# Attention, experts and a product on one core: the softmax division moved from the weights to the outputs, and a different start

## What is computed

```
scores = scale * q @ k.T ;  cum = cumsum(max(s, 0))
scores = where(causal, -1e9, scores + min(-(cum_i - cum_j), 0))
attn   = exp(scores - max(scores))
attn   = attn / (sum(attn) + 1e-9)
x      = attn @ v                       # then 1152 tokens x 512
```

## Time and profile before

| what | value |
|---|---|
| median of 3 runs | 1173.54 us (1171.92 to 1175.3) |
| the profiled execution, its own time | 1174.52 us |
| its span in the trace | 1172.7 us |
| TensorE busy over the span | 98%, 6152 matmuls |
| DVE, ACT, POOL busy | 35%, 24%, 10% |
| mean granted TensorE clock | 0.997 |

### The profile page before, as it was taken

The page is one execution under the profiler, slowest core; times in us unless marked ns, Lnnn a source line. Parts: engine busy times, 40 slices in busy tenths (PEclk is TensorE's granted clock), DMA queues, the critical chain, the costliest instruction groups (busy, mean ns, idle before and its releaser), DMA issues.

```text
span 1172.7 us, 15312 instructions
## 1 busy us (share of the span) xinstructions
PE 1148.6 (98%) x6152; PEld 1029.0 (88%) x6152; DVE 411.5 (35%) x819; ACT 282.2 (24%) x569; POOL 113.0 (10%) x104
## 2 busy tenths in 40 slices
PE   7888899999999999999999999999999999999998
PEld 4666788899989989998998998999899899999997
DVE  4766435332224133232322413322232333433422
ACT  2666321212203112121220312212031231232210
POOL 1998530000000000000000000000000000000000
PEclk9999899999999999999999999999999999999999
DMA  7454220111011021011102202101120120120001
GB/s 195 112 123 102 82 73 1 54 54 36 19 54 72 0 72 59 12 36 54 54 0 72 72 0 70 51 22 34 38 72 1 36 72 1 36 73 10 27 27 54
DMA packets 52537, 59.59 MB, mean 51 GB/s; under 512 B 31600, under 2 KB 31600, under 8 KB 52496
## 3 DMA queue, kind: packets, MB, share of 16 engines
q1 hardware_dynamic: 52496, 59.02, 16.8%
HBM read 56.61 MB, written 2.40 MB: 50 GB/s over the span
## 4 chain that ended last, share of the span: by engine, by line
PE 93%; DVE 3%; ACT 2%; issue 1%; SPq 0%; DMA 0%; DVEq 0%; ACTq 0%
PE bank L1130 16%; PE bank L1132 16%; PE bank L1131 16%; PE bank L1265 13%; PE bank L1267 13%; PE bank L1266 13%; PE bank L1115 2%; DVE pT L740 1%; ACT scores L480 1%; PE bank L1041 1%; DVE scores L696 1%; PE bank L1037 1%; PE bank L1096 1%; PE bank L1002 1%; PE bank L1204 1%
## 5 line engine op out<-in xcount | busy, mean ns | idle before, releaser
L1130 PE MATMUL bank<-xh,w1h 128*128 128x384 f32 x1056 | 354.9, 336 | 0.0
L1132 PE MATMUL bank<-xh,w1l 128*128 128x384 f32 x1056 | 353.2, 334 | 0.0
L1131 PE MATMUL bank<-xl,w1h 128*128 128x384 f32 x1056 | 353.2, 334 | 0.0
L1265 PE MATMUL bank<-w2h,hh 128*128 128x512 f32 x684 | 267.2, 391 | 0.0
L1267 PE MATMUL bank<-w2h,hl 128*128 128x512 f32 x684 | 266.5, 390 | 0.0
L1266 PE MATMUL bank<-w2l,hh 128*128 128x512 f32 x684 | 266.4, 389 | 0.0
L548 ACT ACTIVATE hh<-bank 128x384 fp32r<-128x384 f32 x192 | 94.4, 492 | 618.8 <-PE bank L1132 618.8
L1130 PEld LDWEIGHTS bank<-xh,w1h 128*128 128x128 f32 x1056 | 198.4, 188 | 1.1
L1131 PEld LDWEIGHTS bank<-xl,w1h 128*128 128x128 f32 x1056 | 198.5, 188 | 0.7
L1132 PEld LDWEIGHTS bank<-xh,w1l 128*128 128x128 f32 x1056 | 198.4, 188 | 0.0
L753 DVE SCALAR_TENSOR_TENSOR hl<-bank,hh 128x384 fp32r<-128x384 f32 x192 | 106.7, 556 | 246.8 <-ACT hh L548 246.8
(11 more groups left out here) (107 smaller groups left out, 558.4 us busy)
## 6 DMA issues: line engine op xcount, KB each, us to landing
stage<-in_moe_w SPq DMA_DIRECT2D x64, 512.0 KB, 3.5
bias<-cum_dram SPq DMA_DIRECT2D x14, 288.0 KB, 3.6
stage<-in_moe_w_a SPq DMA_DIRECT2D x12, 256.0 KB, 2.6
stage<-in_moe_w_b SPq DMA_DIRECT2D x12, 256.0 KB, 3.0
stage<-in_moe_w_out SPq DMA_DIRECT2D x12, 256.0 KB, 2.6
bias_tail<-cum_dram SPq DMA_DIRECT2D x16, 144.0 KB, 4.1
nat<-in_q SPq DMA_DIRECT2D x16, 128.0 KB, 3.9
nat<-in_k SPq DMA_DIRECT2D x16, 128.0 KB, 3.2
```

The source lines that it names most:

```text
L1130: pe.matmul(o, w1h[:, c, col:col + PART], high, start=(c == 0), stop=False)
L1131: pe.matmul(o, w1h[:, c, col:col + PART], low, start=False, stop=False)
L1132: ins = pe.matmul(o, w1l[:, c, col:col + PART], high, start=False, stop=(c == KC - 1))
L1265: pe.matmul(o, hh[:, n % 2, f, at], w2h[:, f, :], start=(f == 0), stop=False)
```

## The change

1. POOL no longer multiplies the exponentials. `transpose_p` waits for `exp_done`, not `norm_done`, so unnormalised weights are transposed and multiplied by v.
2. `add_eps` and `invert` run once per pair on all nine columns. `spread_recips(p-1, part)` then spreads the reciprocals on TensorE: it takes a column of them, broadcast to 64 columns, as the weights and the identity as the moving operand, into a bank of the ring. Part 0 (4 matmuls of 128 columns) stands after units 2 and 3 and ahead of `score(p, 2)`; part 1 (4 of 128, 2 of 64) stands after units 5 and 6 and ahead of `score(p+1, 0)`. `copy_spread` (ACT) copies it to `spread`.
3. `scale_x` (DVE) multiplies the attention output by `spread` into `scaled`; `high_x` (ACT) now copies from `scaled`, and `low_x` moves to POOL.
4. `RING` has the two new users, one after unit 3 and one after unit 6.
5. Pair 0's bias is made once, by two matmuls of 512 columns before `score(0, 0)`, and copied by ACT to `bias[0]`; the 8 bias matmuls inside `score_tiles` go, and its memset on POOL too.
6. Pair 0's keys are issued by ScalarE's queue, not SyncE's. Constants are made with fewer waits on DVE, and those that the mask needs are made after `cum_rows`. TensorE runs seven extra matmuls of `own_half` first. `bias` rows are loaded to 512 columns, not 576.

The core of the diff:

```diff
     for _p in range(PAIRS):
         RING += [("unit", _p, u) for u in range(4)]
+        RING.append(("spread", _p, 0))
         if _p + 2 < PAIRS:
             RING.append(("tail", _p + 2))
-        RING += [("unit", _p, u) for u in range(4, 8)]
+        RING += [("unit", _p, u) for u in range(4, 7)]
+        RING.append(("spread", _p, 1))
+        RING.append(("unit", _p, 7))
...
         sp.dma_start(s_rows[:, :], sf).then_inc(s_loaded, DMA)
-        load_qk(0)
+        load_nat(0, qf, 0, q_loaded)
         load_qk(1)
...
-            for t in range(3):
-                normalise(p, t)
+            if p > 0:
+                low_x(p - 1, 0)
...
+        def copy_spread(p, part):
+            lo, hi = QRANGE[part]
+            act.wait_ge(spread_mm, 2 * p + part + 1)
+            at_least(act, x_scaled, 2 * (p - 2) + part + 1)
+            copy(spread[p % 2][:, lo:hi], ring_bank("spread", p, part)[:, 0:hi - lo], spread_done)
+
         def high_x(p, g):
             lo, hi = QRANGE[g]
-            act.wait_ge(pv_mm[g], p + 1)
-            copy(xh[:, p * S + lo:p * S + hi], X_BANK[g][:, 0:hi - lo], x_hi)
+            act.wait_ge(x_scaled, 2 * p + g + 1)
+            copy(xh[:, p * S + lo:p * S + hi], scaled[:, lo:hi], x_hi)
...
                 copy_pT(p - 1, 3)
+                copy_spread(p - 1, 0)
...
                 copy_pT(p - 1, 5)
+                copy_spread(p - 1, 1)
                 copy_pT(p - 1, 7)
...
+        def scale_x(p, g):
+
             lo, hi = QRANGE[g]
-            dve.wait_ge(x_hi, 2 * p + g + 1)
+            dve.wait_ge(pv_mm[g], p + 1)
+            dve.wait_ge(spread_done, 2 * p + g + 1)
+            at_least(dve, x_lo, 2 * (p - 1) + g + 1)
+            dve.tensor_tensor(scaled[:, lo:hi], X_BANK[g][:, 0:hi - lo], spread[p % 2][:, lo:hi],
+                              ALU.mult).then_inc(x_scaled, 1)
...
-                if p == 0:
-                    for r in range(2):
-                        pe.matmul(S_BANK[first + r][:, col:col + n],
-                                  ident[0:HEADS, r:r + 1].broadcast_to([HEADS, PART]), cum_rows[:, 0:n],
-                                  start=False, stop=False)
...
+        def spread_recips(p, part):
+
+            z = p % 2
+            ring_free("spread", p, part)
+            bank = ring_bank("spread", p, part)
+            pe.wait_ge(rec_done, p + 1)
+            for n, t in enumerate((2 * part, 2 * part + 1)):
+                for r in range(2):
+                    c = column(t, r)
+                    ins = pe.matmul(bank[r * D:(r + 1) * D, n * PART:(n + 1) * PART],
+                                    recips[:, z, c:c + 1].broadcast_to([PART, D]), ident[:, :], start=True, stop=True)
...
+            ins.then_inc(spread_mm, 1)
...
+        pe.wait_ge(half_set, 4)
+        for i in range(WARM_UP):
+            pe.matmul(S_BANK[0][:, 0:PART], own_half[:, :], own_half[:, :], start=True, stop=True)
         pe.wait_ge(const_set, 1)
         for i in range(3):
             transpose_qk(0, i)
+        pe.wait_ge(cum_done, 1)
+        for r in range(2):
+            pe.matmul(S_BANK[2 + r][:, :], ident[0:HEADS, r:r + 1].broadcast_to([HEADS, PART]), cum_rows[:, 0:MAIN],
+                      start=True, stop=True).then_inc(first_bias_mm, 1)
         score(0, 0)
...
                 transpose_p(p - 1, 2)
                 transpose_p(p - 1, 3)
+                spread_recips(p - 1, 0)
             score(p, 2)
...
                 transpose_p(p - 1, 5)
                 transpose_p(p - 1, 6)
+                spread_recips(p - 1, 1)
             if not last:
                 score(p + 1, 0)
```

More of the change, by code:

```diff
@@ L25 @@
 SINKHORN_ROUNDS = 8
+WARM_UP = 7
 DMA = 16
@@ L91, in attention_experts_product @@
     small, _ = sb("small", [PART, 96], F32)
-    s_rows, _ = sb("s_rows", [HEADS, S], F32)
+    cum_rows, _ = sb("cum_rows", [HEADS, S], F32)
+    s_rows, at = sb("s_rows", [HEADS, S], F32)
     s_pos, _ = sb("s_pos", [HEADS, S], F32)
-    cum_rows, _ = sb("cum_rows", [HEADS, S], F32)
     zero_rows, _ = sb("zero_rows", [HEADS, S], F32)
+    scaled, at = sb("scaled", [PART, S], F32, at - 4 * S)
+    spread = [None] * 2
+    for z in range(2):
+        spread[z], at = sb(f"spread_{z}", [PART, S], F32, at)
     identb, _ = sb("identb", [PART, PART], BF16)
@@ L409, in spread_tail_queries, with low_x @@
                                ALU.mult).then_inc(bd_done, 1)
-        def normalise(p, t):
-            z = p % 2
-            for r in range(2):
[L414 to L422, removed]
+        def low_x(p, g):
+            lo, hi = QRANGE[g]
+            pool.wait_ge(x_hi, 2 * p + g + 1)
+            cols = slice(p * S + lo, p * S + hi)
+            pool.tensor_tensor(xl[:, cols], scaled[:, lo:hi], xh[:, cols].bitcast(F32), ALU.subtract).then_inc(x_lo, 1)
         def split_w1_first(i):
@@ L510, in _ @@
             high_qk(0, i)
+        for r in range(2):
+            act.wait_ge(first_bias_mm, r + 1)
+            copy(bias[0][:, r, :], S_BANK[2 + r][:, :], first_bias)
         for p in range(PAIRS):
             if p > 1:
-                act.wait_ge(eps_done, 2 * (p - 2) + 2)
+                act.wait_ge(eps_done, p - 1)
             exp_tile(p, 0, 0, 1)
@@ L679, in _ @@
                           ALU.mult).then_inc(cum_done, 1)
+        dve.tensor_scalar(identb[:, :], ramp[:, :], place_of[:, 0:1], None, ALU.is_equal).then_inc(const_set, 1)
+        dve.tensor_scalar(maskb[:, :], ramp[:, :], place_of[:, 0:1], MASKED, ALU.is_gt, ALU.mult).then_inc(const_set, 1)
+        dve.wait_ge(const_set, 3)
+        for r in range(2):
+            rows = slice(r * D, (r + 1) * D)
+            dve.tensor_copy(maskt[rows, :], maskb[rows, r * TAIL:(r + 1) * TAIL]).then_inc(const_set, 1)
         def low_qk(p, i):
@@ L1020, in ring_free @@
                 pe.wait_ge(tr_lo, 3 * p + 3)
+            elif kind == "spread":
+                pe.wait_ge(spread_done, 2 * p + u[0] + 1)
             elif u[0] in BY_DVE:
@@ L1097, in transpose_p @@
             ins.then_inc(pt_mm, 1)
+        def spread_recips(p, part):
[4 more added lines that the diff above has]
+            for n, t in enumerate((2 * part, 2 * part + 1)):
+                for r in range(2):
+                    c = column(t, r)
+                    ins = pe.matmul(bank[r * D:(r + 1) * D, n * PART:(n + 1) * PART],
+                                    recips[:, z, c:c + 1].broadcast_to([PART, D]), ident[:, :], start=True, stop=True)
+            if part == 1:
+                for r in range(2):
+                    rows = slice(r * D, (r + 1) * D)
+                    ins = pe.matmul(bank[rows, 2 * PART:2 * PART + TAIL],
+                                    recips[rows, z, TAIL_COLUMN:TAIL_COLUMN + 1].broadcast_to([D, D]),
+                                    ident[rows, rows], start=True, stop=True)
+            ins.then_inc(spread_mm, 1)
         def attend(p, g):
@@ L1185, in _ @@
         transpose_p(LAST, 3)
+        spread_recips(LAST, 0)
         hidden(0, 0, 2)
@@ L1191, in _ @@
         transpose_p(LAST, 6)
+        spread_recips(LAST, 1)
         hidden(0, 0, 4)
```

110 lines of the change are left out of this document (55 added, 55 removed).

## The result

| what | before | after |
|---|---|---|
| median | 1173.59 us (1171.92 to 1175.3, 4 runs) | 1210.21 us (1206.97 to 1211.98, 4 runs) |
| the profiled execution, its own time | 1174.52 us | 1206.97 us |
| its span | 1172.7 us | 1205.0 us |
| mean granted TensorE clock | 0.997 | 0.984 |

The ratio is 1.0309, with a 95% interval of 1.0282 to 1.0335: the change makes the kernel 36.6 us slower. The forecast was 1198, within 1180 to 1214.

What follows compares the result with a forecast made beforehand. The prediction took a loop of latencies over TensorE, ScalarE and VectorE, not GpSimd, as the bound before the change. Six iterations +27.0, last iteration and last pair +4.8, start -7.5: +24.3 us, giving 1198 us, range 1180 to 1214.

Steps and rivals of the forecast that it cites:

- The loop of latencies: Pair loop over TensorE, ScalarE and VectorE, not GpSimd: added work is paid in full, +4.5 us per iteration, period 18.7.
- the first place: First spreading, ahead of score(p, 2), waits for VectorE's copy of unit 2: +2.0 us more per iteration.
- Both waits: Ahead of each spreading: VectorE's copy of unit 2 adds +2.0 us, ScalarE's copy of unit 5 adds +2.4, per iteration.
- The start of the iteration: VectorE's multiply ahead of ScalarE's copy makes the copy of the next queries late: +0.3 us per iteration.
- the clock falls: Rival: in the loop a longer stretch without other matmuls drops TensorE's clock, 3 to 4 us per iteration; chance 0.19.
- The start: Before the loop: fewer bias matmuls (-6.2), keys sooner and shorter constants (-1.3), -7.5 us; at most 2 beyond.
- The -1.3 (0 to -2): At the start: keys and later SyncE loads come sooner, VectorE's constants are shorter; -1.3 us, between 0 and -2.
- The last iteration and the last pair: Loop's last iteration +1.5 us for spreading and a copy, last pair +1.9 and +1.4 at its two spreadings; +4.8 together.
- between the places: Between the two spreadings: VectorE's multiply needs no wait for `xh` before the split of the tails; -0.2 us per iteration.
- The third: Rival: GpSimd held the loop through `transpose_p`'s wait for normalised tiles, so the change is faster, 1169 or 1163 us; chance 0.15.
- The second: Rival: only one of the loop's two waits is paid, +2.3 us per iteration, 1185 us; chance 0.09.
- The fourth: Rival: the effects cancel, iterations at about +0.5 us, total 1173 us; chance 0.04.

Runs made afterwards that it cites:

- e5_filled: The changed kernel with 6 and 7 matmuls that nobody reads put into TensorE's two waits ahead of the spreading; 1197.64 us, ratio 1.0202.
- h1_start_only: The kernel before with points 5 and 6 of the change and nothing else; 1169.96 us, ratio 0.9965.
- h3_one_queue: `h2_start_loads` with the first keys issued on SyncE's queue again, as before; 1165.61 us, ratio 0.9924.
- e3_second_behind: The changed kernel with only the second spreading group moved behind score(p+1, 0) inside the pair loop; 1191.53 us, ratio 1.0152.
- e1_both_behind: The changed kernel with both spreading groups moved behind the scores they stood ahead of, inside the pair loop only; 1178.39 us, ratio 1.0037.
- e2_first_behind: The changed kernel with only the first spreading group moved behind score(p, 2) inside the pair loop; 1198.51 us, ratio 1.0215.
- e4_no_spread: The changed kernel without spreading matmuls and their copies, the outputs multiplied by ones, so the division is left out; 1167.69 us, ratio 0.9937.
- h2_start_loads: `h1_start_only` with pair 2's queries and keys loaded ahead of w1; 1165.11 us, ratio 0.9929.
- v2_late_loads: The changed kernel, first spreading behind score(p, 2) and copied by VectorE, second behind unit 7 (also in RING), pair 2's loads early; 1168.66 us, ratio 0.9959.
- h4_no_extra: `h2_start_loads` without the extra matmuls at the start (WARM_UP = 0); 1165.59 us, ratio 0.9924.

## Why the prediction came out as it did

**The loop of latencies: right, and shown.** The period at full clock is 18.42 (`e5_filled`), forecast 18.7. That two iterations of the changed kernel took 18.64 and 18.83 is no closer hit: each has a fall of the clock at the first place. From the start of the score there to VectorE's tile 3 they take 1.44 and 1.62 (115.38 to 116.82, 54.16 to 55.78), where the third iteration takes 1.23 (72.98 to 74.21), and these 0.2 and 0.4 are what they have above 18.42. Both waits stand where they were said to: 1.47 ahead of the first spreading, released by VectorE's copy (forecast 1.5), 1.77 ahead of the second, released by ScalarE's (1.8); VectorE's gap ahead of tile 3 is 1.87 (2). The spreading took 0.66 (0.7) and 0.85 from the first to the score behind it (1.0); by columns, the lower bounds of 0.58 and 0.73 were nearer than those by count. The experiments that move each group give 1.55 and 1.23 for the order alone.

**The start of the iteration: +0.3 was too much.** The product's output waits for VectorE, and ScalarE's copy of the queries starts 0.9 after it as forecast, but an iteration with the multiply and without the spreading is 0.1 longer. The two errors in the loop, 0.3 for 0.1 and 1.0 for 0.85, make up most of the 0.3 between 18.7 and 18.42.

**What was mis-sized: the clock.** The prediction took "the clock falls" as a rival that would replace the forecast, at 3 to 4 in each iteration that has it, 1205 for two and 1219 for six. It came in all six. The prediction named "the clock column shows 0.5 to 0.8 in every iteration" as a sign of being wrong, and it came true: around the six falls the column reads 0.60 (40 to 45), 0.71 (53 to 57), 0.62 (80 to 88), 0.51 (103 to 109.4), 0.66 (115 to 120) and 0.71 (142 to 147.8). What kept the total near is the price: the six iterations lost 10.8 to it in the profiled execution (0.2 to 3.3 each), not 21, since a fall at the first place costs 0.2 to 0.4 and one at the second lasted for only a part of the product in the sixth iteration (3.39, not 4.32). The median's 1210 lies between the rival's two numbers. The clock is worth 12.6 in the medians. The step that failed is the choice of a likeliest case without any fall, worth 12.6 that the sum has at nothing, though the rows of the last iteration showed one behind a stretch of the same making, only longer.

**The rest agrees partly by luck.** `e5_filled` ran in 1197.64 and the forecast was 1198, but its terms are not those of the sum. From the kernel before to `e5_filled` the spans grew by 22.0: the six iterations +25.2 (forecast 27.0), the last iteration and the last pair +1.7 (forecast 4.8), the earlier start of the first iteration -5.0 (forecast -7.5). The cost was put too high and the gain too high as well, and the two errors cancel in part.

**The start: -7.5 was -4.1**, as `h1_start_only` measures it alone (in the changed kernel the first iteration starts 5.2 earlier). The sum of what was removed was a little low (pair 1's first bias comes 8.5 earlier, forecast 7 to 8). The bound on it was put wrongly: the forecast let pair 2's keys cap the gain at 2 beyond 7.5; it is pair 2's queries that cap it, and below 7.5. The -1.3 (0 to -2) for the keys' queue and the constants has no sign of the queue in it: `h3_one_queue` runs without it in the same time.

**The last iteration and the last pair: +4.8 was +1.4.** The last pair gave +2.9 (forecast 3.3). The last iteration gave -1.5 (forecast +1.5), and two things are seen in it. Its product ran at full speed here (159.45 to 161.66), which is 2.1 less. The spreading stands in the stretch where the clock had fallen before, but that it kept the clock up is not shown: `e3_second_behind` has the same order of matmuls there and its product took 3.71, while `e1_both_behind` and `e2_first_behind` had 2.27. So the 2.1 may be luck of this execution. And VectorE no longer waits for `xh`: the forecast's -0.2 "between the places" is all of the wait there, since no split of tails stands behind it. In the kernel before, and in `e4_no_spread`:

```profile
123.63 0.42 DVE L746 TENSOR_TENSOR xl<-bank,xh 128x256 fp32r<-128x256 f32 x1 [1.16 <-ACT xh L464]
```

```profile
118.30 0.42 DVE L766 TENSOR_TENSOR scaled<-bank,spread 128x256 f32<-128x256 f32 x1
```

`e4_no_spread`, which does the same start as `h1_start_only`, is 2.3 faster than it in the medians. In the two profiled executions, 1.2 apart, its last iteration takes 12.55 against 14.50, with products of nearly the same length (3.52 and 3.68), and no other part gains more than 0.4.

**The rivals.** The third, that GpSimd held the loop, falls with `e4_no_spread`. The second, that only one wait is paid, falls with `e2_first_behind` and `e3_second_behind`, which add. The fourth falls with the result. The first, the falling clock, is what happened, beside the waits of the forecast and not in place of them.

**A step ahead of the start that stays open.** The forecast gave the extra matmuls no effect. It also named a rule of the Trainium skill, "TensorE: Matmul & The Clock Gate", section "What's actually happening", that activity releases the throttle, by which they could have one. In the changed kernel the bias matmuls took 3.77, as before, so there the rule is not borne out. In `h2_start_loads`, with the same extra matmuls, the transposes at 6.18 took 1.06 for eight records instead of 1.94, and the bias matmuls 2.65, as the rule would have it; then the clock fell:

```profile
6.00:8.00 2.00, 1.82 (x12) 1.37 (x13) 1.48 (x6) 1.16 (x3) 0.00 (x0) 1.00 0.77 167
8.00:10.00 2.00, 2.00 (x4) 0.34 (x2) 0.96 (x3) 0.70 (x2) 0.72 (x1) 0.65 0.60 137
10.00:12.00 2.00, 2.00 (x15) 1.56 (x14) 0.00 (x0) 0.60 (x1) 0.00 (x0) 0.50 0.70 172
```

So the same start runs in two ways, and the early speed was lost again on the way. Of the eleven kernels profiled with the extra matmuls, four ran fast there (bias matmuls of 2.38 to 2.65 in `e5_filled`, `h2_start_loads`, `h3_one_queue` and `v2_late_loads`) and seven took 3.77 to 3.78, as did `h4_no_extra`, which has none. Over the runs it is worth nothing (1165.59 without). What decides which of the two it is was not settled.

## What to carry to other kernels

Before giving idle engines less to do, see whether anything waits for them: an engine at 10 of 10 us whose period stays the same at 7.6 of 10 is not the bound, and work put elsewhere to relieve it is paid on the loop that is. In an in-order engine the place of a wait costs more than the instruction: the moved division with its ten matmuls costs 4.2 us per iteration with them ahead of the scores, 1.4 behind them, and 0.5 in the best order found, and a ring of buffers decides which copy they wait for. If an added wait lengthens a stretch in which TensorE does little, count the clock in as a part of the sum, not as another case; matmuls that nobody reads can be cheaper than the fall.

## What the runs showed of the hardware

- Iterations with the same instructions see the clock fall at different points and for different lengths: in `e2_first_behind` the same product took 4.32, 3.23, 3.99, 4.32, 2.28 and 2.28 in six of them in a row, and in the changed kernel the fall met the product in four of six (3.39 to 4.32) and the score at the first place in two.
- The clock fell while TensorE was counted busy for the whole window: 0.65 and then 0.50 from 8 to 12 us of `h2_start_loads`, during and behind the four records (2.65 us) of the bias matmuls with 16 rows.
- The granted clock reads 1.00 up to 20 us in the changed kernel, where TensorE's matmuls took twice as long as later: 1.06 for four transposes at 14.45 against 0.61 at 50.28. At the start of a trace the durations tell more than that column.
- With six and seven added matmuls in the two waits the clock read 1.00 from 30 us to the end of the loop of `e5_filled`, and its iterations were 18.42 to 18.45, under the 18.64 and 18.83 of the two iterations of the changed kernel whose product ran at full speed.
- With the keys' load issued through a second queue at the same time as the queries', the first transposes of the queries started at 6.18 instead of 4.68 us, and those of the keys right behind them, about when they did with one queue (6.44).
